# The attention bias moves from TensorE to VectorE's pass for the minimum, and the transposes one round further behind the scores

## The reference, cut to what matters

```python
B, H, S, D = 4, 8, 576, 64                  # q, k, v: float32
scores = (q @ k.transpose(0, 1, 3, 2)) / sqrt(D)
rel = pos[:, None] - pos[None, :]
slopes = 2.0 ** (-8.0 * (arange(H) + 1) / H)
bias = slopes[:, None, None] * -abs(rel)
mask = (rel >= 0) & (rel < 128)
scores = where(mask, scores + bias[None], -1e9)
scores = scores - max(scores, axis=-1, keepdims=True)
attn = exp(scores)
attn = attn / (sum(attn, axis=-1, keepdims=True) + 1e-09)
out = attn @ v                              # (B, H, S, D)
x = out.transpose(0, 2, 1, 3).reshape(B * S, H * D)
x = experts(x)        # skip test, argmax gate over 8 experts, relu layer, x + gate * y
out = feed_forward(x) # h = x @ w_in; (h * tanh(softplus(h))) @ w_out
```

## Time and profile before

| | |
|---|---|
| median of 3 runs | 784.52 us (782.53 to 785.69) |
| the profiled execution | 783.5 us, its span 781.7 us |
| PE busy | 764.8 us (98%) |
| DVE busy | 516.5 us (66%) |
| ACT busy | 366.2 us (47%) |
| POOL busy | 109.4 us (14%) |
| granted TensorE clock, mean | 0.991 |
| attention, first to last product | 1.45 us to 168.5 us |
| transfers in the span | 78.22 MB, mean 100 GB/s |

### The profile page before, as it was taken

The page is one execution under the profiler, slowest core; times in us unless marked ns, Lnnn a source line. Parts: engine busy times, 40 slices in busy tenths (PEclk is TensorE's granted clock), DMA queues, the critical chain, the costliest instruction groups (busy, mean ns, idle before and its releaser), DMA issues.

```text
span 781.7 us, 13724 instructions
## 1 busy us (share of the span) xinstructions
PE 764.8 (98%) x4652; PEld 586.8 (75%) x4652; DVE 516.5 (66%) x1138; ACT 366.2 (47%) x885; POOL 109.4 (14%) x254
## 2 busy tenths in 40 slices
PE   8999999998999999999999999999999999999998
PEld 5788888876333333338889989898989898989886
DVE  4667676774111111337998888888878888888885
ACT  5677777730111011442655545464555455545544
POOL 3555555511111020000000000000000000000000
PEclk8999999998999999999999999999999999999999
DMA  6666898612978185004001101010110001001001
GB/s 224 196 182 205 273 285 285 211 31 49 339 288 310 37 303 204 8 16 140 1 2 41 41 0 42 1 41 2 40 41 0 27 14 40 0 0 41 1 1 41
DMA packets 53052, 78.22 MB, mean 100 GB/s; under 512 B 24548, under 2 KB 26212, under 8 KB 52961
## 3 DMA queue, kind: packets, MB, share of 16 engines
q1 hardware_dynamic: 50944, 72.02, 28.1%
q0 software_dynamic: 1600, 4.85, 1.7%
q10 hardware_dynamic: 432, 0.41, 0.2%
HBM read 65.53 MB, written 12.56 MB: 100 GB/s over the span
## 4 chain that ended last, share of the span: by engine, by line
PE 87%; DVE 4%; DMA 3%; issue 2%; ACT 2%; POOLq 0%; POOL 0%; ACTq 0%; SPq 0%; DVEq 0%
PE ps_y L1433 16%; PE ps_xt L1416 12%; PE ps_ht L1416 12%; PE ps_y L1123 9%; PE ps_h L1433 8%; PE ps_h L1105 8%; PE ps_out_t L578 5%; PE ps_probs_t L561 5%; PE ps_scores L550 4%; PE ps_x L589 4%; PE ps_scores L534 2%; DMA x_in<-tokens,job_entry 1%; PE ps_h L1402 1%; DVE h_sb L1015 1%; DMA k_raw<-in_kT 1%
## 5 line engine op out<-in xcount | busy, mean ns | idle before, releaser
L1305 ACT ACTIVATE u_sb<-u_sb 128x384 f32<-128x384 f32 x96 | 50.6, 527 | 105.3 <-DVE u_sb L1353 105.3
L1309 ACT ACTIVATE r_sb<-n_sb,all_consts 128x384 f32<-128x384 f32 x96 | 59.3, 617 | 85.3 <-DVE n_sb L1369 85.3
L382 ACT ACTIVATE probs<-ps_scores,neg_max 128x256 f32<-128x256 f32 (+2 forms) x160 | 66.5, 426 | 30.0 <-DVE neg_max L434 30.0
L1433 PE MATMUL ps_y<-ffn_lo,g_hi 128*128 128x512 f32 x192 | 76.6, 399 | 0.0
L1433 PE MATMUL ps_y<-ffn_hi,g_lo 128*128 128x512 f32 x192 | 75.9, 396 | 0.0
L1433 PE MATMUL ps_y<-ffn_hi,g_hi 128*128 128x512 f32 x192 | 75.7, 395 | 0.0
L434 DVE TENSOR_REDUCE neg_max<-ps_scores 128x1 f32<-128x256 f32 (+2 forms) x160 | 48.6, 362 | 31.7 <-PE ps_scores L550 31.5
L1416 PE MATMUL ps_xt<-xt_hi,ffn_lo 128*128 128x384 f32 x192 | 66.1, 344 | 0.8 <-DVE xt_lo L1344 0.8
L1381 DVE SCALAR_TENSOR_TENSOR u_sb<-n_sb,r_sb 128x384 f32<-128x384 f32 x96 | 53.7, 559 | 19.1 <-ACT r_sb L1311 19.1
L1416 PE MATMUL ps_ht<-xt_hi,ffn_lo 128*128 128x384 f32 x192 | 66.0, 344 | 0.0
L1416 PE MATMUL ps_xt<-xt_hi,ffn_hi 128*128 128x384 f32 x192 | 64.9, 338 | 0.0
(11 more groups left out here) (179 smaller groups left out, 1633.1 us busy)
## 6 DMA issues: line engine op xcount, KB each, us to landing
experts_even<-in_w SPq DMA_DIRECT2D x8, 2048.0 KB, 10.9
w_sb<-in_w SPq DMA_DIRECT2D x8, 2048.0 KB, 12.2
ffn_raw<-in_w_ffn SPq DMA_DIRECT2D x16, 512.0 KB, 5.7
q_raw<-in_qT SPq DMA_DIRECT2D x15, 288.0 KB, 3.9
k_raw<-in_kT SPq DMA_DIRECT2D x15, 288.0 KB, 4.5
v_sb<-in_v SPq DMA_DIRECT2D x16, 256.0 KB, 2.7
tokens<-x_out SPq DMA_DIRECT2D x64, 64.0 KB, 3.7
x_sb<-tokens SPq DMA_DIRECT2D x5, 768.0 KB, 4.5
```

What stands on the lines that cost most here:

```text
L382: nc.scalar.activation(probs[0:n, r, h, 0:w], ps_scores[t.ring][0:n, h, 0:w], ACT.Exp, bias=neg_max[0:n, r, h:h + 1], scale=-1.0, accum_ou ...
L1305: nc.scalar.activation(u_sb[:, t.r], u_sb[:, t.r], ACT.Exp).then_inc(u_ready, 1)
L1309: nc.scalar.activation(r_sb[:, t.r], n_sb[:, t.f % NB], ACT.Ln, bias=cst["two"]).then_inc(ln_ready, 1)
L1433: m = nc.tensor.matmul(ps_o[i][:, :], a[:, t.r, P * i:P * i + P], ffn[b][:, at:at + D], start=(t.f == 0 and n == 0), stop=(t.f == FT - 1 a ...
```

## The change

The bias is no longer multiplied in by PE. DVE's pass over the scores becomes one fused instruction per head: it reads `ps_scores` and `bias_sb`, adds them, writes the sum to `probs` in SBUF and gives the minimum as accumulator output. ACT's exp then reads `probs` and writes in place. `bias_sb` is plain float32 and is loaded directly; the rounding copies on ACT and POOL, `bias_raw`, `ident_r` and the waits for them go. `scores` now starts the accumulation, and waits for the minimum of the tile two back where `add_bias` waited for its exps. The ring of `probs` has 8 tiles. Transposes, values and their copies come two rounds behind the scores (`LAG_T`), turning back and scaling three (`LAG_X`). SP issues the load of q and k of pair n+2 ahead of the wait for the values of pair n-1.

```diff
+    RING_P = 8
+    LAG_T = 2
+    LAG_X = 3
-    bias_raw = nc.alloc_sbuf_tensor_at("bias_raw", [P, HP, 2, 2 * P], F32, offset=ffn["free"])
-    bias_sb = sb("bias_sb", [P, HP, 2, 2 * P], F32R)
-    ident_r = sb("ident_r", [P, P], F32R)
-    probs = sb("probs", [P, 4, 2, 2 * P])
+    bias_sb = sb("bias_sb", [P, HP, 2, 2 * P])
+    probs = sb("probs", [P, RING_P, 2, 2 * P])
-    neg_max = sb("neg_max", [P, 4, 2])
+    neg_max = sb("neg_max", [P, RING_P, 2])
...
     def load_experts(i):
-            if i == 0:
-                sp.wait_ge(bias_first, 1)
-                sp.wait_ge(bias_ready, HP - 1)
...
         for n in range(PAIRS):
+            if n + 1 < HP:
+                load_bias(n + 1)
+            if n + 2 < PAIRS:
+                sp.wait_ge(q_lo_ready, n + 1)
+                sp.wait_ge(k_lo_ready, n + 1)
+                load_qk(n + 2)
             if n + 1 < PAIRS:
                 if n >= 1:
                     sp.wait_ge(out_t_ready, n * QT)
                 load_v(n + 1)
-                if n + 1 < HP:
-                    load_bias(n + 1)
-            if n + 2 < PAIRS:
-                sp.wait_ge(q_lo_ready, n + 1)
-                sp.wait_ge(k_lo_ready, n + 1)
-                load_qk(n + 2)
...
     # POOL
-        nc.gpsimd.tensor_copy(ident_r[:], ident).then_inc(ident_ready, 1)
-                    if t.i == 3 and t.pair < HP - 1:
-                        make_bias(t.pair + 1)
-            if r >= 3:
-                for t in tiles_of(r - 3):
+            if r > LAG_X:
+                for t in tiles_of(r - LAG_X - 1):
                     copy_gate(t)
...
     # ACT, exps(t)
-            if t.k >= 4:
-                act.wait_ge(probs_t_ready, t.k - 3)
-                nc.scalar.activation(probs[0:n, r, h, 0:w], ps_scores[t.ring][0:n, h, 0:w], ACT.Exp,
+                nc.scalar.activation(probs[0:n, r, h, 0:w], probs[0:n, r, h, 0:w], ACT.Exp,
...
-        act.wait_ge(bias_loaded[0], 16)
-        nc.scalar.activation(bias_sb[:, 0], bias_raw[:, 0], ACT.Copy).then_inc(bias_first, 1)
...
-            if r >= 1:
-                copy_probs_t(Stage(2 * r - 1))
+            if r >= LAG_T:
+                copy_probs_t(tiles_of(r - LAG_T)[1])
...
     # DVE, find_max(t)
-            if t.k >= 4:
-                dve.wait_ge(probs_ready, 2 * t.k - 6)
+            if t.pair < HP and t.i == 0:
+                dve.wait_ge(bias_loaded[t.hp], 16)
+            if t.k >= RING_P:
+                dve.wait_ge(probs_t_ready, t.k - RING_P + 1)
             for h in range(2):
-                nc.vector.tensor_reduce(neg_max[0:n, r, h:h + 1], ps_scores[t.ring][0:n, h, 0:w], AX_X,
-                                        ALU.min).then_inc(max_ready, 1)
+                nc.vector.tensor_tensor_reduce(
+                    probs[0:n, r, h, 0:w], ps_scores[t.ring][0:n, h, 0:w], bias_sb[0:n, t.hp, h, b0:b1],
+                    1.0, BIG, ALU.add, ALU.min, neg_max[0:n, r, h:h + 1]).then_inc(max_ready, 1)
...
     # DVE, the loop over rounds: copy_probs_t and copy_out_t of r - LAG_T, invert and scale_x of r - LAG_X
...
     # PE
-        def add_bias(t):
-            if t.k >= 2:
-                pe.wait_ge(probs_ready, 2 * t.k - 2)
-            for h in range(2):
-                nc.tensor.matmul(ps_scores[t.ring][0:n, h, 0:w], ident_r[:, 0:n], bias_sb[:, t.hp, h, b0:b1],
-                                 start=True, stop=False)
         def scores(t):
+            if t.k >= 2:
+                pe.wait_ge(max_ready, 2 * t.k - 2)
...
-                                         start=False, stop=(step == 2))
+                                         start=(step == 0), stop=(step == 2))
...
-        for r in range(ROUNDS + 2):
-            if 1 <= r <= ROUNDS:
-                for t in tiles_of(r - 1):
+        for r in range(ROUNDS + LAG_X):
+            if LAG_T <= r < ROUNDS + LAG_T:
+                for t in tiles_of(r - LAG_T):
                     transpose_probs(t)
             if r < ROUNDS:
                 for t in tiles_of(r):
-                    add_bias(t)
-                for t in tiles_of(r):
                     scores(t)
-            if 1 <= r <= ROUNDS:
-                for t in tiles_of(r - 1):
+            if LAG_T <= r < ROUNDS + LAG_T:
+                for t in tiles_of(r - LAG_T):
                     times_values(t)
-            if r >= 2:
-                for t in tiles_of(r - 2):
+            if r >= LAG_X:
+                for t in tiles_of(r - LAG_X):
                     turn_back(t)
```

More of the change, by code:

```diff
@@ L159, in attention @@
     qk_first_ready = sem("qk_first_ready")
-    bias_first = sem("bias_first")
     bias_loaded = [sem(f"bias_loaded{hp}") for hp in range(HP)]
@@ L196, in __init__ @@
             self.n = rows(self.i)
-            self.ring, self.ring4 = k % 2, k % 4
+            self.ring, self.ring_p = k % 2, k % RING_P
             self.slot = self.pair % 2
@@ L244, in load_bias @@
         def load_bias(hp):
-            sp.dma_start(bias_raw[:, hp], dram["bias"][hp]).then_inc(bias_loaded[hp], 16)
+            sp.dma_start(bias_sb[:, hp], dram["bias"][hp]).then_inc(bias_loaded[hp], 16)
         def load_weights(n):
@@ L345, in _ @@
         make_k(1)
-        for r in range(ROUNDS + 3):
+        for r in range(ROUNDS + LAG_X + 1):
             if r < ROUNDS:
@@ L373, in exps @@
         def exps(t):
-            r, n = t.ring4, t.n
+            r, n = t.ring_p, t.n
             w = keys(t.i)[1] - keys(t.i)[0]
-            if t.k >= 4:
-                act.wait_ge(probs_t_ready, t.k - 3)
             if t.k >= RING_S:
@@ L408, in _ @@
         nc.scalar.activation(k_hi[:, 0, 0:FIRST], first, ACT.Copy).then_inc(first_k_hi, 1)
-        act.wait_ge(bias_loaded[0], 16)
-        nc.scalar.activation(bias_sb[:, 0], bias_raw[:, 0], ACT.Copy).then_inc(bias_first, 1)
         scale_k(0)
-        for r in range(ROUNDS + 1):
-            if r >= 1:
-                copy_probs_t(Stage(2 * r - 1))
+        for r in range(ROUNDS + LAG_T):
+            if r >= LAG_T:
+                copy_probs_t(tiles_of(r - LAG_T)[1])
             if r < ROUNDS:
@@ L476, in scale_x @@
                 inv_sums[:, r % 2].unsqueeze(3).broadcast_to([P, 2, 2, DH + GE]), ALU.mult).then_inc(x_scaled, 1)
-        nc.vector.memset(probs[:, 0], 1.0).then_inc(warm_ready, 1)
+        nc.vector.memset(probs[:, RING_P - 1], 1.0).then_inc(warm_ready, 1)
         nc.vector.memset(sums_eps[:], 1.0).then_inc(eps_set, 1)
@@ L504, in add_logits @@
                                     ).then_inc(cst["logits_added"], 1)
-        for r in range(ROUNDS + 2):
-            if r % (HP * QT // 2) == 5 and r > HP * QT // 2:
+        for r in range(ROUNDS + LAG_X):
+            if r % (HP * QT // 2) == 6 and r > HP * QT // 2:
                 add_logits(r // (HP * QT // 2) - 1)
-            if 1 <= r <= ROUNDS:
-                copy_probs_t(Stage(2 * r - 2))
+            if LAG_T <= r < ROUNDS + LAG_T:
+                copy_probs_t(tiles_of(r - LAG_T)[0])
             if r < ROUNDS:
@@ L515, in _ @@
                 rest_of_k()
-            if 1 <= r <= ROUNDS:
-                copy_out_t(r - 1)
-            if r >= 2:
-                invert(r - 2)
-                scale_x(r - 2)
+            if LAG_T <= r < ROUNDS + LAG_T:
+                copy_out_t(r - LAG_T)
+            if r >= LAG_X:
+                invert(r - LAG_X)
+                scale_x(r - LAG_X)
         add_logits(B - 1)
@@ L524, in _ @@
     def _(pe):
-        def add_bias(t):
-            n, w = t.n, keys(t.i)[1] - keys(t.i)[0]
-            b0, b1 = bias_columns(t.i)
-            if t.pair < HP and t.i == 0:
-                pe.wait_ge(*((bias_ready, t.hp) if t.hp else (bias_first, 1)))
-            if t.k >= 2:
-                pe.wait_ge(probs_ready, 2 * t.k - 2)
-            for h in range(2):
-                nc.tensor.matmul(ps_scores[t.ring][0:n, h, 0:w], ident_r[:, 0:n], bias_sb[:, t.hp, h, b0:b1],
-                                 start=True, stop=False)
         def scores(t):
@@ L560, in transpose_probs @@
                 for c, (_, size, at) in enumerate(blocks(t.i)):
-                    m = nc.tensor.transpose(ps_probs_t[r][0:size, c, h, 0:n], probs[0:n, t.ring4, h, at:at + size],
+                    m = nc.tensor.transpose(ps_probs_t[r][0:size, c, h, 0:n], probs[0:n, t.ring_p, h, at:at + size],
                                             ident[0:n, 0:n])
@@ L592, in _ @@
         pe.wait_ge(warm_ready, 1)
-        ones = probs[:, 0].rearrange("p h c -> p (h c)")
+        ones = probs[:, RING_P - 1].rearrange("p h c -> p (h c)")
         for _ in range(WARM):
@@ L596, in _ @@
         pe.wait_ge(cst["loaded"], 16)
-        pe.wait_ge(ident_ready, 1)
-        for r in range(ROUNDS + 2):
-            if 1 <= r <= ROUNDS:
-                for t in tiles_of(r - 1):
+        for r in range(ROUNDS + LAG_X):
+            if LAG_T <= r < ROUNDS + LAG_T:
+                for t in tiles_of(r - LAG_T):
                     transpose_probs(t)
```

13 lines of the change are left out of this document (4 added, 9 removed).

## The result

The changed kernel takes 772.8 us (median of 4 runs, 770.95 to 774.79) against 783.7 us of the kernel before beside it (782.53 to 785.69, 4 runs): ratio 0.9859, 95% interval 0.9825 to 0.9893. That is 1.4% faster; forecast were 769.5 us, in a range of 763.5 to 781. The profiled execution took 770.95 us (span 768.8), which is the fastest of the four; the one before took 783.5 (span 781.7). The difference to be explained in the traces is 12.9 us of span, where the sum said 14.5.

A forecast was written before the change was run, and what follows sets the result against it. Attention was taken as bound by PE's own work, 3.88 us a round. Terms 3.2 + 16.6 + 0.5 - 3.3 - 1.5 - 1.0 = 14.5 us less than 783.5 gave 769.0, set at 769.5 us; range 763.5 to 781.

The forecast's parts named there:

- The bias products: PE in attention: removing them saves 0.462 us a round, 2.31 us in five rounds; lower end 1.8 us.
- the rival of the refilled slot: PE's switch from transposes to scores costs what the bias products hid; 775 us, up to 781; chance 0.04.
- DVE's instruction: DVE's fused bias and minimum: a main instruction and an overlapped accumulator read, adding 0.09 us, between 0 and 0.23.
- d: What the fused DVE instruction adds to the plain minimum's 0.33 us between starts; taken as 0.09 us.
- The rival of the half rate: DVE's fused pass runs at half rate and bounds the kernel: 796 us; DVE bound and slower had chance 0.09.
- DVE's room: DVE needs 14.85 of 17.1 us in five rounds without the 20 fused instructions' additions, leaving 0.11 us for each.
- ACT reads SBUF: ACT's exps from SBUF take 0.04 us more each, 0.8 us in five rounds; ends 0 and 0.05.
- The stall behind `scale_k`: ACT's copy of the odd tile comes late behind two activations of 0.68 us: 1 us over 14 pairs, ends 0 and 3.
- SP's queue: Rival: k load behind a 2 MB load just fits; if not, ACT and POOL wait, 5 us lost, 774; chance 0.07.
- the 14.6 of rounds 4 to 39: Gain in these attention rounds: 16.6 + 0.5 for the wait - 1.5 DVE stalls - 1.0 ACT stalls, in us.
- The start: Start of attention: round 4 begins 3.2 us ahead, PE's clock at its lower level; not about 3 us means wrong.
- The end: End of attention: last scaling about 8.0 us after round 38's transposes start, 3.3 us later than before.

The follow-up runs named there:

- e2: Kernel before, bias products kept on PE, with the new lag, ring of 8 and SP load order: ratio to before 1.0028, 786.3 us.
- e6: Changed kernel with the `scale_k` of a round's odd tile moved to the next round, behind the copy and ahead of the exps: 772.1 us, ratio 0.9861.
- e8: Changed kernel with `scale_k` of the odd tile a round later and experts' loads of 1 MB per pair: 767.4 us, ratio to before 0.9804.
- e1: Changed kernel with LAG_T = 1 and LAG_X = 2, so the fused bias alone: 770.4 us, ratio to before 0.9828.
- e9: Changed kernel with an added DVE minimum over 64 columns of constants behind each fused instruction: 775.7 us, ratio to before 0.9907.
- e10: Changed kernel with an added DVE minimum over 128 columns of constants behind each fused instruction: 778.6 us, ratio to before 0.9909.
- e5: The changed kernel once more, unaltered: 774.9 us, ratio to before 0.9884.
- e3: Changed kernel with two PE products per tile of the bias products' size added, overwritten by the scores: 795.4 us, ratio to before 1.0132.
- e4: Changed kernel with SP's loads in the old order, v and bias ahead of q and k: 802.8 us, ratio to before 1.0223.

## Why the prediction was right, and where its terms were off

- **The bias products.** Put at 2.31 us in five rounds, with a lower end of 1.8 if the switch remained. With the lag in both, e2 against e6 and e8 gives 19.13 - 16.69 = 2.44, with one round of lag e1 gives 1.91 and a wait for exps beside it. The whole share of the chain was there to be had; the rival of the refilled slot fell.
- **DVE's instruction.** The kind was right (two instructions, overlapped), the size not: d is 0.015 and not 0.09, since the next instruction starts together with the read, where on ACT it starts 0.10 us after it. The rival of the half rate fell with it: 0.345 us for 256 columns, where it would have been 0.60. By the Trainium skill's sentence that an op that writes out its accumulator is two instructions ("VectorE: DVE Perf Modes", section "Two Vector instructions with no wait between them"), the trace agrees, with a read of 84 ns. The Trainium skill's sentence that a scalar-tensor-tensor op halves its throughput with two float32 sources in SBUF ("Vector Engine (DVE) Microarchitecture Reference", section "Points that are easy to get wrong") doesn't bear on this form, which has one source in PSUM; its reason, applied all the same, would have halved the rate, and the 0.345 us show the full one.
- **DVE's room.** Put at 0.11 us; e9 and e10 show more. In e10 five rounds are 17.61 us and not 14.85 + 20 x 0.21 = 19.05. Of these 1.44 us, 0.54 are the 1.3 us that x_out waits for the reciprocal, which I called time that nothing gives back: DVE is busy for 16.85 of the 17.61 us, so only 0.76 is left of all its waits. Another 0.40 are the share of the sum of logits, which falls in neither window. The last 0.5 are busy time: 13.15 (the 13.95 of the earlier trace rows without that sum) + 20 x 0.21 would be 17.35 and not 16.85. That wasn't taken apart, but in e10's timeline each instruction starts some 0.07 us before the one ahead of it ends (47.26 against 46.91 + 0.42), and this overlap comes only where no wait stands between. The weight loads' waits for DVE's copy in the changed kernel were 1.0 us, where 1.5 stood for PE.
- **ACT reads SBUF.** Put at 0.04 us more an exp; now they start 44.66 - 44.16 = 0.50 us apart, 0.45 before, and ACT's busy time rose by 0.75 us in five rounds, where 0.8 stood. The stall behind `scale_k` was named with its mechanism and put at 1 us; it is 0.36 x 7 = 2.5 us, shown by e6 and e8.
- **SP's queue.** Held to be a rival at 0.07 that "just fits". It did not: ACT waited 6.9 us in four places for k. The load of k went out 6.5 us after the experts' load, as counted, but landed at 13.6 and not by 11 to 13, and ACT wanted it at 11.2 to 12.1 and not at 13.0. One part of the 13.0 that failed is the 2.1 us by which the experts' load was to go out sooner once q and k no longer stand ahead of it: from the load of v to it are 92.55 - 89.41 = 3.1 us in the kernel before and 1.5 to 2.4 in the changed one, so 0.8 to 1.6 us. Between rounds 5 and 40 the periods hold 3.8 us over seven times 17.04, nearly all of it in the four that have a late k (0.9, 0.1, 1.3 and 1.5 us). The term was missing from the sum; it was put at 5 us with a chance of 0.07, and its chance was the error more than its price.
- **Why the sum still met the 14.6 of rounds 4 to 39.** From the start of round 5 (27.57 before, 21.39 after) to that of round 40 it is 136.30 - 123.12 = 13.2 us: seven times 19.40 - 16.68 = 2.72 makes 19.0, and 0.5 of the bias wait; less 2.5 for ACT's order and 3.8 for late loads and DVE. The bare round was better than forecast (3.34 us and not 3.42) and the stalls were 6.3 and not 2.5; two errors that cancel. So the mechanism was right, but that 17.1 and 14.6 were met so closely is luck.
- **The start.** 4.9 us ahead, not 3.2. The steps were in the order counted, but the granted clock was low for 3.4 us and not for 6.8 as before, which is worth 1.7 us. The prediction kept the low level until 17.5 us. It had named a start that isn't about 3 us ahead as a sign of being wrong; by this sign the start was missed, and on the good side by luck: e5, the same kernel, had 10.2 us of low clock there and was at 20.73 in round 4.
- **The end.** Last scaling at +8.05 us, forecast +8.0.
- **What follows attention** gave back 3.1 us, for which no term stood. Two places in the chain hold 2.8 of it: 1.47 us in which PE waits for nothing that the profile shows, behind the first pair of the second experts' weights, and the load of `x_sb`, 5.08 us here and 3.77 before.

```profile
208.57 1.47 issue
```
```profile
342.62 5.08 DMA x_sb<-tokens
```

The load took 2.85 to 5.49 us over the other runs, whatever was changed (4.94 in e5, 5.49 in e3), so this is scatter. The wait at 208.57 was 0 in the kernel before, in e2 and in e3, and 0.7 to 1.8 us in all other runs. So it came with the change: the three without it are those in which PE still issues products of the bias's size. A shorter attention doesn't explain it, since e4's ends later than that of the kernel before and e4 has the wait (1.2 us). No run took it apart, and it stays open.

- **The median** is 2 us above the profiled execution. Its granted clock was 0.993 in the mean, that of the other three 0.985 to 0.991; e5 shows what one late load and the clock behind it can cost.

## What to carry to other kernels

Before work goes from the bound engine to another, measure the pitch of the new instruction and not its duration: here a two-input pass with an accumulator output took DVE 0.42 us, but only 0.015 us more of its time than the plain minimum. When the bound engine gets faster, every load whose time was set by its round is wanted sooner: work out for each the time from issue to use, and split the large transfers ahead of it: with halves of 1 MB ACT's waits for k fell from 6.9 to 1.1 us. A longer software pipeline is paid once at its end, and it has to save more in the rounds than it costs there and in what it makes late. Here the extra round brought nothing by itself (e1), and by the periods it did so only once the other stalls were gone (e8).

## What the runs showed of the hardware that I had not expected

- An accumulator read on DVE takes 84 ns, and the next main instruction starts with it: both at 43.98, and the pitch is 0.345 us, where the plain minimum's is 0.33.
- Where PE had stood idle, spells at a granted clock of 0.50 followed that lasted 3.4, 6.8 or 10.2 us: at the start (3.4 us in the changed kernel, 6.8 before, 10.2 in e5), after the routing table (6.8 us), and in mid-attention in e5 (10.2 us, after 1.9 us with next to no product) and in e4. Two executions of the same kernel differ in which of them they get.
- In e3 two products over all of the array's rows cost 0.23 us behind transposes and 0.44 behind products over half the rows.
- The exp of a 128x256 head starts every 0.50 us where it reads SBUF and writes in place, and every 0.45 us where it reads PSUM and writes SBUF; which of the two differences costs the 0.05 us isn't shown.
